# The projection's tiles one quarter of a unit sooner, and another order in units 0 and 1

## The reference, cut to what matters

```python
def _attn_ref(q, k, v, a_re, a_im):                 # B=4, H=8, S=768, D=48
    mag = np.sqrt(a_re * a_re + a_im * a_im)
    scale = np.minimum(mag, 0.999) / (mag + 1e-06)
    a_re_n, a_im_n = (a_re * scale, a_im * scale)
    for t in range(S):
        ar, ai = (a_re_n[:, :, t, :, None], a_im_n[:, :, t, :, None])
        new_re, new_im = ar * S_re - ai * S_im, ar * S_im + ai * S_re
        S_re, S_im = (new_re + k_t outer v_t, new_im)
        y[:, :, t] = np.einsum('bhd,bhde->bhe', q[:, :, t], S_re)

def _moe_ref(x, w_in, w_out):                       # x: 3072 x 384, d_ff = 2048
    h = x @ w_in
    g = np.where(h >= 1, h, np.where(h <= -1, 0.0, (h + 1) ** 2 / 4.0))
    return g @ w_out

def _moe2_ref(x, w_gate, w1, w2):                   # 8 experts, d_ff = 1024
    P = gate(x @ w_gate)                            # exp, then 8 rounds of row and column sums
    for e in range(E):
        out += P[:, e:e + 1] * (np.maximum(x @ w1[e], 0.0) @ w2[e])
```

## Time and profile before

| | |
|---|---|
| median of 3 runs | 2300.43 us (2298.07 to 2301.52) |
| the profiled execution | 2298.59 us, its span 2296.8 us |
| TensorE clock granted, mean | 0.994 of full |
| PE busy | 2226.7 us, 97% of the span |
| DVE busy | 1733.0 us, 75% |
| ACT busy | 1006.9 us, 44% |
| POOL busy | 465.5 us, 20% |
| chain that ended last | PE 90%, DVE 8%, issue 1%, ACT 1% |

### The profile page before, as it was taken

One profiled execution on the slowest core, in us unless ns is written; L12 is line 12 of the kernel. 1 busy time (PEld: TensorE's weight loads), 2 busy tenths in 40 slices (PEclk: granted clock), 3 DMA queues, 4 the chain that ended last, 5 costly groups with the idle time before them and its releaser, 6 DMA issues.

```text
span 2296.8 us, 37984 instructions
## 1 busy us (share of the span) xinstructions
PE 2226.7 (97%) x13699; PEld 2075.5 (90%) x13699; DVE 1733.0 (75%) x3049; ACT 1006.9 (44%) x1702; POOL 465.5 (20%) x310
## 2 busy tenths in 40 slices
PE   3899999999999899999999999999999999999999
PEld 3799999999999789999998899999998999999998
DVE  7898888888855867767778777777778777777775
ACT  3566666566555423343334333343333433344332
POOL 0000000000000422322323222332232222232222
PEclk9899999999999999999999999999999999999999
DMA  3311111111103031111111231011110211111111
GB/s 109 94 52 53 52 50 50 50 50 50 43 29 138 28 111 37 47 55 55 55 39 44 83 111 54 29 55 55 55 55 28 83 56 56 43 40 55 55 55 28
DMA packets 70725, 131.33 MB, mean 57 GB/s; under 512 B 5512, under 2 KB 36488, under 8 KB 70536
## 3 DMA queue, kind: packets, MB, share of 16 engines
q1 hardware_dynamic: 70536, 129.14, 17.4%
HBM read 114.96 MB, written 14.16 MB: 56 GB/s over the span
## 4 chain that ended last, share of the span: by engine, by line
PE 90%; DVE 8%; issue 1%; ACT 1%; DMA 0%; SPq 0%; DVEq 0%; ACTq 0%
PE bank L1547 16%; PE bank L1548 15%; PE bank L1549 15%; PE bank L1730 11%; PE bank L1732 11%; PE bank L1731 11%; PE bank L1527 2%; PE bank L1528 2%; PE bank L1518 1%; PE bank L1534 1%; PE bank L1493 1%; DVE tmp L947 1%; PE bank L1477 1%; DVE u_s L1334 0%; PE bank L1488 0%
## 5 line engine op out<-in xcount | busy, mean ns | idle before, releaser
L606 POOL TENSOR_TENSOR h_l<-u_s,h_h 128x512 fp32r<-128x512 f32 x192 | 245.0, 1298 | 1618.8 <-ACT h_h L854 1618.8
L1730 PE MATMUL bank<-w_h,h_h 128*128 128x384 f32 x1536 | 515.9, 336 | 11.1 <-DVE acc L1360 6.8
L1732 PE MATMUL bank<-w_h,h_l 128*128 128x384 f32 x1536 | 514.1, 335 | 0.0
L1731 PE MATMUL bank<-w_l,h_h 128*128 128x384 f32 x1536 | 514.0, 335 | 0.0
L1548 PE MATMUL bank<-x_l,w_h 128*128 128x512 f32 x1056 | 414.2, 392 | 0.0
L1547 PE MATMUL bank<-x_h,w_h 128*128 128x512 f32 x1056 | 414.0, 392 | 0.0
L1549 PE MATMUL bank<-x_h,w_l 128*128 128x512 f32 x1056 | 413.2, 391 | 0.0
L1360 DVE SCALAR_TENSOR_TENSOR acc<-bank,prob,acc 128x384 f32<-128x384 f32 x352 | 214.6, 612 | 174.3 <-PE bank L1732 171.5
L1730 PEld LDWEIGHTS bank<-w_h,h_h 128*128 128x128 f32 x1536 | 288.7, 188 | 16.8 <-DVE acc L1360 9.6
L1731 PEld LDWEIGHTS bank<-w_l,h_h 128*128 128x128 f32 x1536 | 288.8, 188 | 2.0
L1732 PEld LDWEIGHTS bank<-w_h,h_l 128*128 128x128 f32 x1536 | 288.7, 188 | 0.0
(11 more groups left out here) (188 smaller groups left out, 3976.1 us busy)
## 6 DMA issues: line engine op xcount, KB each, us to landing
stage<-w_ SPq DMA_DIRECT2D x48, 768.0 KB, 6.6
w_raw<-w_ SPq DMA_DIRECT2D x96, 384.0 KB, 3.6
qb<-q_in_ SPq DMA_DIRECT2D x24, 192.0 KB
kb<-k_in_ SPq DMA_DIRECT2D x24, 192.0 KB
vb<-v_in_ SPq DMA_DIRECT2D x24, 192.0 KB
x_hi<-x2h_s SPq DMA_DIRECT2D x36, 128.0 KB, 1.8
x_lo<-x2l_s SPq DMA_DIRECT2D x36, 128.0 KB, 1.8
x_h<-x_hi SPq DMA_DIRECT2D x3, 1536.0 KB, 10.5
```

Of the source, the lines that this page charges most:

```text
L606: pool.tensor_tensor(tiles_of(h_l, name), group_sum(name), tiles_of(h_h, name).bitcast(F32), ALU.subtract).then_inc(hl_done, 1)
L1730: pe.matmul(dst, h_h[:, f, t_], w2h[:, fw], start=n == 0, stop=False)
L1731: pe.matmul(dst, h_h[:, f, t_], w2l[:, fw], start=False, stop=False)
L1732: mm = pe.matmul(dst, h_l[:, f, t_], w2h[:, fw], start=False, stop=n == 3)
```

## The change

All steps of the tiles in `unit(u)`, on PE, ACT and DVE, go by t = 4(u - 2) instead of 4(u - 2) - 1. So unit 2 has tiles 0 to 3 instead of 0 to 2, and the tail begins with tile 88 instead of 87. In unit 2 mm_in(0) stands ahead of p_by_tokens. x2_hi and x2_lo stand one tile step earlier in their unit: x2_hi ahead of p_root, x2_lo right behind the masks.

In units 0 and 1: masked(0) stands ahead of scale(2). PE makes the differences of pieces 0 and 1 behind r_by_tokens(1) instead of at the end of unit 0. DVE does k_by_r(1) and by_k(1) ahead of the first block step, and the masks of unit 1 after four block steps instead of seven; state_add(1) stands in the middle of the scan, x_lo(1) ahead of its last step. ACT does p_sq(2) behind the low parts of pieces 4 and 5. The table of pieces starts one slot sooner, and waits on pieces are set for mm_in(0) and mm_out(0), as they use the banks of the differences.

```diff
@@ ACT and PE, unit(u); DVE the same @@
-                t = 4 * (u - 2) - 1
+                t = 4 * (u - 2)
@@ ACT, unit(u) @@
                 tile_hi(t)
                 tile_sq(t + 1)
 
+                if even and u >= 4:
+                    x2_hi(u // 2 - 2)
                 if even:
                     p_root(u + 1)
...
-                if even and u >= 4:
-                    x2_hi(u // 2 - 2)
                 tile_hi(t + 2)
...
                 y_out(u)
-                if not even and more:
+                if not even and more and u > 1:
                     p_sq(u + 1)
                 x_hi(u)
                 if u == 1:
                     first_lo(4, BY_PE)
+                    p_sq(2)
@@ DVE, first_unit and second_unit @@
                 p_sum(1)
+                masked(0)
                 scale(2)
-                masked(0)
...
                 by_q(1)
-                blocks(1, 1, 2)
                 k_by_r(1)
                 by_k(1)
-                blocks(1, 2, NI)
+                blocks(1, 1, 5)
                 masked(1)
+                blocks(1, 5, NI)
                 scan_init(1)
-                scan(1, 0, 4)
+                scan(1, 0, 2)
                 state_add(1)
+                scan(1, 2, 3)
+                x_lo(1)
+                scan(1, 3, 4)
                 final(2)
-                x_lo(1)
...
-            FIRST_LO = {2: ((), (6, 7), (7, 8), (8, 10)), 3: ((10, 11), (11, 12), (12, 13), (13, 14)),
-                        4: ((14, 15), (15, 16), (), ())}
+            FIRST_LO = {2: ((6, 7), (7, 8), (), (8, 11)), 3: ((11, 12), (12, 13), (13, 14), (14, 15)),
+                        4: ((15, 16), (), (), ())}
@@ DVE, unit(u) @@
                 masked(u)
+                if even and u >= 4:
+                    x2_lo(u // 2 - 2)
                 tile_max(t + 1)
...
                 tile_max(t + 2)
-                if even and u >= 4:
-                    x2_lo(u // 2 - 2)
@@ all three, the tail @@
-            for m in range(-1, TILES):
+            for m in range(TILES):
@@ PE, mm_in and mm_out @@
-                    pe.wait_ge(piece_l, PIECES.index((0, m)) + 1)
+                    pe.wait_ge(piece_l, PIECES.index((0, m)) + 1 if m else BY_PE - 1)
...
-                    pe.wait_ge(piece_l, PIECES.index((1, m)) + 1)
+                    pe.wait_ge(piece_l, PIECES.index((1, m)) + 1 if m else BY_PE)
@@ PE, the units @@
+                if u == 2:
+                    mm_in(0)
                 p_by_tokens(u)
-                tile_in(t)
+                if u != 2:
+                    tile_in(t)
                 r_by_tokens(u)
+                if u == 1:
+                    first_lo(0, 2)
...
-                if u < 2:
-                    first_lo(4 * u, 4 * u + 2)
+                if u == 1:
+                    first_lo(4, BY_PE)
```

More of the change, by code:

```diff
@@ L1295, in _ @@
                 unit(u)
-            g_max((GROUPS - 1) * TILES - 2)
-            for m in range(-1, TILES):
+            g_max((GROUPS - 1) * TILES - 1)
+            for m in range(TILES):
                 t = (GROUPS - 1) * TILES + m
```

## The result

The changed kernel takes 2302.78 us (median of 20 runs, 2300.17 to 2305.49), the kernel before 2299.93 (20 runs, 2297.80 to 2301.52). The ratio is 1.0016, with a 95% interval from 1.0010 to 1.0022: 2.3 to 5.1 us slower. The bound of 4.6 us that I had set between "the same" and "slower" lies within that. Forecast were 2304.9 us, and +4.5 us against the kernel before. The profiled execution of after took 2303.65 us (span 2301.8), against 2298.59 (span 2296.8) before.

The account below looks back on a forecast made before the run. PE was taken to bound from 220 to 720 us, VectorE to set the pace before 112 us and in units 3 and 4. Terms -4.24 + 0.2 + 1.9 + 6.6 = +4.5 gave 2304.9 us in median terms; range 2298.0 to 2308.5.

Parts of the forecast that it names:

- The moved tile: Tail behind unit 23: one tile fewer there, its mm_in moved to unit 2 where PE idles: -4.24 us.
- The loads behind the tail: Next stage's loads, issued at the end of unit 23: some 6 us of cover left, cost 0, at most 4.24.
- The start: Units 0 to 4, paced by DVE: the new orders bring r of unit 4 +0.2 us, bounds -2.3 and +1.6.
- rival A: Pieces of unit 1: clock high through both, all to unit 4 shifts by 2.5 us: +2.0, 2302.4; chance 0.17.
- Rival B: Pieces of unit 1: clock low until both are done, q transposes 1.4 us later: +5.9, 2306.3; chance 0.20.
- nothing beyond the tile: Start to unit 4: the new orders only make room for the moved tile; +0.2 us at r of unit 4.
- The new wait of VectorE: Unit 1: DVE waits 2.0 us before state_add(1) for PE's state sum.
- The cover of x_lo: A new group's mm_in waits for x_lo one mm_in sooner; in unit 10, 1.4 us of cover, cost 0.
- The even units: Units 6 to 20: PE waits 0.83 us for x2_lo before a group's first mm_out, eight times: +6.6 us.
- Unit 4: PE's mm_out waits 2.2 us for x2_lo, a present 0.31 us wait goes: +1.9 us.
- C: Even units: waits don't come, as DVE gains 0.83 us on PE before the masks: -2.1, 2298.3; chance 0.10.
- D: No even-unit waits plus a high clock or larger gain at the start: -4.6 and below, 2295.8; chance 0.08.

Follow-up runs that it names:

- after's second trace: The changed kernel run once more, without any further edit, for one more trace: 2301.93 us.
- x2_lo one later: Changed kernel with x2_lo behind tile_max(t + 1) on VectorE in the even units from 4 on: 2313.62 us, ratio 1.0066 to the kernel before.
- the edit to x2_lo: Changed kernel with x2_lo on VectorE ahead of the masks in the even units from 4 on: 2294.72 us, ratio 0.9980 to the kernel before.

## Why the prediction was right, point by point

The range held the time, and the median came 2.1 us under the forecast. Of that, 0.5 us is the kernel before, whose median was 2299.93 in the comparison and 2300.43 in the runs I had; the rest is, by the terms below, the start, whose clock is high in a part of the traces. Of its parts:

**The moved tile, -4.24**: from r of unit 23 to the nought matmul of the last group it took 38.88 us before and 34.64 after: -4.24. The loads behind the tail kept their cover: their first reader on VectorE starts at 722.82 us in after, with no idle time before it.

**The start, +0.2 at r of unit 4**: the working behind the q transposes was exact, the clock ahead of them was a spread. I took the pieces' end at 60.6 (58.8 to 62); the eight traces with the start as changed have 58.13 to 60.63, four of them below 58.5 and so under my lower bound. From there to r of unit 2 I had 23.25 us, and the traces have 23.24 or 23.25. From r of unit 2 to r of unit 4 I had 58.05, and the seven of these traces that have the shift show 57.93 to 58.03. So r of unit 4 comes at 139.5 where the clock is high (139.3 to 139.7 in three traces; rival A: 139.4) and at 141.1 to 141.8 where it isn't (the forecast: 141.9). Forecast and rival A are both right, in about as many traces, though A's 2.5 us did not follow from my bound: 60.6 - 58.8 is 1.8. Rival B's "low all through" came in none of the eight. The fault in my statement was to treat the clock as one unknown with one answer, where it came out otherwise from run to run. The Trainium skill says in "TensorE: Matmul & The Clock Gate", Part 1 (What's actually happening), that activity releases the slow clock. I took from that that the pieces begin slow after a wait. The traces bear it out in part only. Behind waits of 0.52 us and less the clock stayed at 1.00. In three of the five traces with a wait of 1.88 us and more, r of unit 1 still ran at 1.00 (its first row has 0.39 us, in the other two 0.59), and the clock fell 0.5 to 1 us after PE had gone on.

That the new orders give "nothing beyond the tile" holds against the kernel before where the clock at the pieces is low (r of unit 4 at 141.08 to 141.80, against 141.72), and not where it is high. But under the shift they are needed: with the old orders r of unit 4 stood at 143.49 (table moved), 2.4 us later than the 141.09 of after's second trace.

**The new wait of VectorE, 2.0**: 1.91 us, and worth 1.66 when removed.

**The cover of x_lo, cost 0**: it is there in the even units from 6 on, but I had looked at unit 10 only. In unit 4 the first mm_in of the group waited 0.85 us for x_lo (the third line of the table of waits). It cost 0.2 us at most: r of that unit waits for VectorE's r_last besides, which was done at 139.27 us, and r started at 139.52.

**The even units, 8 x 0.83 = +6.6**: the place, the number and the one-for-one price are right, the size is too large: 8 x 0.67 = +5.4. VectorE's side was exact. From r of unit 10 (308.45 us before) to the masks of the earlier trace rows it took 11.35 us, and it is 322.25 - 310.91 = 11.34:

```profile
310.91 0.28 PE L1489 MATMUL bank<-r_last,ones 128*128 128x4 f32 x2
```

```profile
322.25 0.68 DVE L1062 TENSOR_TENSOR at<-bank,mask 128x512 f32<-128x512 f32 x1
...
323.45 0.68 DVE L1090 TENSOR_TENSOR x2l_s<-bank,x2h_s 128x512 fp32r<-128x512 f32 x1
```

PE's side was not: it reached its mm_out 12.63 us behind r (324.28 - 0.74 - 310.91), where I took 12.47 from the earlier trace rows, with other tiles in between. That takes 0.16 us off the wait; 0.07 us came on top, mostly as PE went on 0.15 us behind the end of x2_lo's first half (323.45 + 0.68), where I took 0.06. That leaves a wait of 0.74, and two units without a wait take 55.40 us in the new order, 0.07 less than before. My bounds of 0.75 to 0.95 per unit missed the 0.67. Unit 22 has no wait, as forecast.

**Unit 4, +1.9**: the wait is 2.17 us (2.2 forecast) and costs 1.7, but in both traces of after the clock was low behind it, and then unit 4 costs 3.24 and 3.30. With x2_lo one later it was low too (3.90, for a wait of 2.83), with the old orders of units 0 and 1 it was not (1.69, for 2.15). This is the step that failed: I priced the wait at its length, though the earlier trace rows show the low clock behind an idle time of 4.3 us, and I used it for unit 1 only. That two errors of opposite sign, 1.3 us here and 1.2 in the even units, nearly cancel is luck.

**The sum**: measured terms with the clock of the first trace are -4.24 - 2.20 + 3.24 + 5.31 = +2.1; with that of the second, 712.45 - 708.93 = +3.5. The interval is 2.3 to 5.1, and the medians differ by 2.85. Rivals C and D of the prediction needed even units without a wait; that took the edit to x2_lo, which then gave what C and D hoped for.

**The second stage.** From the nought matmul of the last group to the end of the span it took 1587.87 us before and 1590.76 in after's first trace, but 1587.65 in its second. Over 13 traces, in which this part of the program is the same, it goes from 1587.65 to 1591.85. Two places make the difference in after's first trace. Behind a wait of 4.22 us at 805 us the clock was low for some 7 us in place of 3.5, which cost 1.3 us. Behind a wait of 1.78 us at 1267 us it was low too, and before it was not behind the same wait. So the 2.9 us of the first trace are not the change's; they are told here as they show how far one trace may lead astray.

## What to carry to other kernels

Where two engines start from the same event and one of them waits for the other a few microseconds on, moving the step that waits (here PE's nought matmul) one place sooner costs the difference in every round. Move the step that it waits for too (here VectorE's x2_lo, ahead of work that has slack), and the gain of the move stays: 2294.7 in place of 2302.8 us. A wait of the bound engine is priced by its length and by a chance of the low clock behind it, which in this kernel cost 1.5 to 1.6 us each time in the units. When tiles move, the table that feeds them has to move too: without it the same shift cost 4.5 us more (in its trace some 1.5 us of that was low clock).

## What the runs showed of the hardware

Behind a wait of PE in a stretch where it is otherwise busy, the granted clock fell to 0.50 in some runs and stayed at 1.00 in others. All waits of 0.7 us and more from 88 us on, in the 13 traces:

| length of the wait, us | waits | with low clock in it or behind it |
|---|---|---|
| 0.7 to 1.25 | 145 | 0 |
| 1.3 to 1.7 | 24 | 3 |
| 1.75 to 1.78 | 26 | 6 |
| 1.98 to 2.34 | 5 | 3 |
| 2.83 and 3.82 | 2 | 2 |
| 4.21 to 4.25 | 13 | 13 |

The three of the second line are the ones before the nought matmul in x2_lo one later. Each low clock behind a wait for x2_lo cost 1.5 to 1.6 us of PE's time.

Up to r of unit 2 the program is the same in the eight traces with the changed start, but for the first tile, which one of them lacks; r of unit 2 comes between 81.38 and 83.87 us. The second stage, whose program is the same in all 13 traces, differs by up to 4.2 us. The stretch between, from r of unit 5 to r of unit 21, repeats to 0.2 us in the two traces of after and to 0.06 us in the three with x2_lo ahead of the masks. And the ten traces suggest, without a run that forces it, that a faster PE can end later: it waits where it was early, and the clock is low when its work is on the path again.
